# Moving the first tile's pairs three slots later in a two-layer TensorE pipeline

## The reference

```python
h = x @ w_in;   g = h * np.cos(h);        x = g @ w_out            # layer 1
h = np.maximum(x @ w_in2, 0.0);           out = (h * h) @ w_out2   # layer 2
```

## Time and profile before

| | us |
|---|---|
| median of 3 runs | 2253.63 (2253.51 to 2253.69) |
| profiled execution, its own time | 2253.41 |
| its span | 2251.1 |
| TensorE busy | 2239.1 (99%) |
| VectorE busy | 1774.6 (79%) |
| ScalarE busy | 1734.8 (77%) |

### The profile page before, as it was taken

The page is one execution under the profiler, slowest core; times in us unless marked ns, Lnnn a source line. Parts: engine busy times, 40 slices in busy tenths (PEclk is TensorE's granted clock), DMA queues, the critical chain, the costliest instruction groups (busy, mean ns, idle before and its releaser), DMA issues.

```text
span 2251.1 us, 46857 instructions
## 1 busy us (share of the span) xinstructions
PE 2239.1 (99%) x19526; PEld 2213.3 (98%) x19526; DVE 1774.6 (79%) x1813; ACT 1734.8 (77%) x1844; POOL 0.2 (0%) x4
## 2 busy tenths in 40 slices
PE   8999999999999999999999999999999999999999
PEld 7899999999999999999999999999999999999998
DVE  8887788777787777887778877778877788777773
ACT  6677777777877777777778777787777787777876
POOL 0000000000000000000000000000000000000000
PEclk9999999999999999999999999999999999999999
DMA  4000000000000000000000000000000000000000
GB/s 127 27 15 15 9 14 12 10 14 7 14 14 7 14 9 13 14 7 14 14 7 14 14 7 14 7 14 14 7 14 14 7 14 14 7 14 7 7 8 15
DMA packets 13456, 33.26 MB, mean 15 GB/s; under 512 B 1905, under 2 KB 1905, under 8 KB 13169
## 3 DMA queue, kind: packets, MB, share of 16 engines
q1 hardware_dynamic: 13280, 32.81, 4.9%
q10 hardware_dynamic: 144, 0.00, 0.0%
HBM read 20.22 MB, written 12.58 MB: 15 GB/s over the span
## 4 chain that ended last, share of the span: by engine, by line
PE 97%; DVE 2%; ACT 1%; issue 0%; DMA 0%
PE h L346 10%; PE h L350 10%; PE h L348 10%; PE h L352 10%; PE y_A L402 5%; PE y_A L396 5%; PE y_A L400 5%; PE y_A L398 5%; PE y_A L404 5%; PE h L355 5%; PE y_B L400 5%; PE y_B L398 5%; PE y_B L396 5%; PE y_B L404 5%; PE y_B L402 5%; DVE conv L712 0%
## 5 line engine op out<-in xcount | busy, mean ns | idle before, releaser
L698 DVE TENSOR_TENSOR g_lo<-g,g_hi 128x1024 fp32r<-128x1024 f32 x512 | 625.2, 1221 | 272.0 <-ACT g_hi L545 271.1
L545 ACT ACTIVATE g_hi<-g 128x1024 fp32r<-128x1024 f32 x512 | 538.3, 1052 | 44.1 <-DVE g L694 43.4
L537 ACT ACTIVATE w<-w,quarter 128x1024 f32<-128x1024 f32 x256 | 295.5, 1154 | 304.6 <-DVE w L688 304.6
L396 PE MATMUL y_A<-g_hi,dn_lo_A 64*128 64x512 f32 x1024 | 396.9, 388 | 0.1
L402 PE MATMUL y_A<-g_hi,dn_side_A 64*128 64x512 f32 x1024 | 396.3, 387 | 0.0
L398 PE MATMUL y_A<-g_hi,dn_hi_A 64*128 64x512 f32 x1024 | 396.0, 387 | 0.0
L400 PE MATMUL y_A<-g_lo,dn_hi_A 64*128 64x512 f32 x1024 | 395.8, 387 | 0.0
L404 PE MATMUL y_A<-g_lo,dn_side_A 64*128 64x512 f32 x1024 | 395.8, 387 | 0.0
L348 PE MATMUL h<-x_hi_A,up_lo_A 64*128 64x512 f32 x1024 | 394.5, 387 | 0.0
L352 PE MATMUL h<-x_hi_A,up_hi_A 64*128 64x512 f32 x1024 | 394.5, 386 | 0.0
L350 PE MATMUL h<-x_lo_A,up_hi_A 64*128 64x512 f32 x1024 | 394.4, 386 | 0.0
(11 more groups left out here) (122 smaller groups left out, 6180.0 us busy)
## 6 DMA issues: line engine op xcount, KB each, us to landing
xt<-x SPq DMA_DIRECT2D x32, 393.0 KB, 3.1
out<-late SPq DMA_DIRECT2D x32, 256.0 KB, 2.0
out<-late SPq DMA_DIRECT2D x32, 128.0 KB, 2.3
late<-w_out SPq DMA_DIRECT2D x2, 1536.0 KB, 9.5
stage_in_side<-w_in SPq DMA_DIRECT2D x2, 512.0 KB, 4.2
stage_in_side<-w_in SPq DMA_DIRECT2D x4, 256.0 KB, 5.3
w<-w_in SPq DMA_DIRECT2D x1, 768.0 KB, 7.1
stage_in_side<-w_in SPq DMA_DIRECT2D x2, 384.0 KB, 9.1
```

The lines of the kernel that those rows point to most:

```text
L396: mm = pe.matmul(sums[:, 0, :], dn_lo[kind][rows, c, :], hi, start=a, stop=False)
L545: act.activation(g_hi[:, s % RING, :, :], g[:, s % RING, :, :], ACT.Copy).then_inc(hi_made[kind], 1)
L698: dve.tensor_tensor(g_lo[:, r, :, :], g[:, r, :, :], g_hi[:, r, :, :].bitcast(F32), ALU.subtract).then_inc(lo_made[kind], 1)
```

## The change

The first tile's A pairs move from slots 3 to 10 of turn 0 to slots 6 to 13. With the lag of four slots, A6 and A7 of the first tile now go down in slots 0 and 1 of turn 1, in the same slots in which A0' and A1' go up. Turn 1 gets its own table: A0', A1', A2' and then B0', where it was A0', A1', B0', A2'. The read of y_A in turn 1 moves from slot 0 to slot 2 on both ScalarE and VectorE. The taps for the second tile move by two slots, so each stands one A pair earlier; the split of its x is done on ScalarE in slot 13 (that of A7) and on VectorE in slot 15. The low parts of the layer-2 weights get new slots, and those of w_out2 are parted. The fill stays with the down step of A5 and of A6. Down steps of turn 0 all wait for the low part before they begin; A6 and A7, now in turn 1, begin with the high part.

```diff
-FIRST_SLOTS = [("B", 0), ("B", 1), ("B", 2), ("A", 0), ("A", 1), ("A", 2), ("A", 3), ("A", 4),
-               ("A", 5), ("A", 6), ("A", 7), ("B", 3), ("B", 4), ("B", 5), ("B", 6), ("B", 7)]
+FIRST_SLOTS = [("B", 0), ("B", 1), ("B", 2), ("B", 3), ("B", 4), ("B", 5), ("A", 0), ("A", 1),
+               ("A", 2), ("A", 3), ("A", 4), ("A", 5), ("A", 6), ("A", 7), ("B", 6), ("B", 7)]
+SECOND_SLOTS = [("A", 0), ("A", 1), ("A", 2), ("B", 0), ("B", 1), ("B", 2), ("A", 3), ("A", 4),
+                ("A", 5), ("A", 6), ("B", 3), ("A", 7), ("B", 4), ("B", 5), ("B", 6), ("B", 7)]
...
-FIRST_TAP_SLOTS = (4, 5, 6, 7, 8, 9, 10)
+FIRST_TAP_SLOTS = (6, 7, 8, 9, 10, 11, 12)
...
-FIRST_SPLIT_SLOTS, FIRST_LOW_SPLIT_SLOT = (12, 12), 13
+FIRST_SPLIT_SLOTS, FIRST_LOW_SPLIT_SLOT = (13, 13), 15
...
-Y1_SLOT, Y2_SLOT = 0, 3
+Y1_SLOT, SECOND_Y1_SLOT, Y2_SLOT = 0, 2, 3
...
-LATE_AT = {(0, 6): 1, (0, 8): 2, (0, 9): 3, (1, 7): 4}
-LATE_LOW_AT = {(0, 14): 1, (1, 2): 2, (1, 9): 3}
+LATE_AT = {(0, 9): 1, (0, 11): 2, (0, 12): 3, (1, 7): 4}
+
+LATE_LOW_AT = {(0, 15): (1, (0, 1)), (1, 0): (2, (1,)), (1, 3): (2, (0,)), (1, 9): (3, (0, 1))}
...
+        if self.peeled and self.i - back == 1:
+            return SECOND_SLOTS
...
+    def y1_slot(self):
+        return SECOND_Y1_SLOT if self.peeled and self.i == 1 else Y1_SLOT
...
-                return turn.peeled and (turn.i == 1 or turn.i == 0 and p == NP - 1)
+                return turn.peeled and turn.i == 1
...
+                    if turn.peeled and turn.i - back == 0 and made == "A" and runs and q in FILL:
+                        on_zeros(FILL[q])
                     if turn.runs(kind) and runs:
                         up_and_down(turn, s, kind, p, down)
...
-                        if turn.peeled and turn.i == 0 and q in FILL:
-                            on_zeros(FILL[q])
                         down_alone(turn, down)
...
-                    if s == Y1_SLOT and turn.runs("A", 1) and turn.slots() is not LAST_SLOTS:
+                    if s == turn.y1_slot() and turn.runs("A", 1) and turn.slots() is not LAST_SLOTS:
                         read_y1(turn, 1)
...
-                for m, (lo, staged, hi) in enumerate(parts):
-
+                for m in parts_of:
+                    lo, staged, hi = parts[m]
```

More of the change, by code:

```diff
@@ L368, in down_waits @@
                     pe.wait_ge(y2_summed, turn.i - 1)
-                if fine(turn, p):
+                if fine(turn):
                     pe.wait_ge(hi_made[kind], turn.count(kind, p, back))
@@ L372, in down_waits, with fine @@
                     pe.wait_ge(lo_made[kind], turn.count(kind, p, back))
-            def fine(turn, p):
-                return turn.peeled and (turn.i == 1 or turn.i == 0 and p == NP - 1)
+            def fine(turn):
+                return turn.peeled and turn.i == 1
             def down_step(turn, r, kind, p, back, rows, k, first, apart=False):
@@ L388, in down_step @@
                 sums = y["B"] if apart and rows is low and k < 6 else layer_out(turn, kind, back)
-                if fine(turn, p) and k in (2, 7):
+                if fine(turn) and k in (2, 7):
                     pe.wait_ge(lo_made[kind], turn.count(kind, p, back))
@@ L664, in layer1_down_lo, with late_lo_part @@
                                          op1=ALU.subtract).then_inc(late_lo, 1)
-            def late_lo_part(n):
+            def late_lo_part(n, parts_of):
                 if n in (1, 3):
@@ L781, in body @@
                     if turn.peeled and (turn.i, s) in LATE_LOW_AT:
-                        late_lo_part(LATE_LOW_AT[turn.i, s])
+                        late_lo_part(*LATE_LOW_AT[turn.i, s])
             turns(dve, body)
```

## The result

| | before | after |
|---|---|---|
| median | 2253.51 (7 runs, 2252.93 to 2253.70) | 2261.53 (7 runs, 2259.87 to 2262.66) |
| profiled execution, its own time | 2253.41 | 2259.87 |
| its span | 2251.1 | 2258.1 |
| granted clock over the span | 0.999 | 0.997 |

The ratio is 1.0035, with a 95% interval of 1.0024 to 1.0047: the change costs 8.0 us. The forecast was 2259.8 in a range of 2257.0 to 2262.2, slower with a chance of 0.81; the median lies inside the range, 1.7 us above the forecast. Note already here that the profiled execution of the changed kernel is the fastest of its seven; the others took 1.2 to 2.8 us more, where all seven of the kernel before lie within 0.8. The slowest, 2262.66, has a span of 2259.7 like the five at 2261.10 to 2261.74 (2259.3 to 2260.0), so its last 1.1 us lie outside the span.

What follows compares the result with a forecast made beforehand. TensorE, busy 99%, was taken as the bound, with a VectorE-ScalarE ring limiting the stretch before slot 4 of turn 1. Schedule 4.5 + clock 1.7 = 6.2 us on 2253.6 gave 2259.8 us, range 2257.0 to 2262.2.

Steps and rivals of the forecast that it cites:

- Part 1: Taps one A pair earlier: tap 0 ahead of A0's fraction makes everything from there to A6's 0.93 us later.
- Part 2: ScalarE's x split between A7's copy and A6's high part: x1_made at 66.3, a new TensorE wait of 2.3 us.
- Part 3: Slots A0'/A6 and A1'/A7 run from 66.4, done at 75.4; the 18.70 row shows two pairs' matmuls starting together.
- Part 4: Read of y_A behind A1's cosine on ScalarE: B0' waits about 4.3 us for x2_made, slot 4 comes 4.5 us later.
- The sum of the schedule: Start of slot 4 in turn 1 against 82.00, without clock loss: 4.5 us later.
- finish line: Start of slot 4 of turn 1, at 82.00 before; its shift prices the change if no new wait follows.
- Part 5: Granted clock behind the new TensorE waits: 1.7 us lost at the second, 0 at the first (bounds 0 and 1.7).
- Rival C: Both new waits cost the clock: 6.2 + 1.7 us, 2261.5 us; chance 0.18.
- Rival B: No clock lost at either new wait: +4.5 us, 2258.1 us; chance 0.16.
- Rival D: Pairing works, y_A read once A7 is down, B0' input ready: line at 81.2, 2252.8 us; chance 0.11, 0.03 faster.
- milder case: Read of y_A at once at 75.4: x2_made at 78.9, start of slot 4 at 82.4, time 2254.0 us.
- Rival E: VectorE's ring stays behind after slot 4, adding up to 1.5 us: 2261.3 us; chance 0.05.

Runs made afterwards that it cites:

- the read first: Changed kernel with the read and split of y_A one slot earlier (slot 1 of turn 1): 2256.64 us; with zeros in the remaining pauses as well, 2255.29 us.
- the filled kernel: Changed kernel with 16 matmuls on zeros ahead of B0' going up in turn 1 and 16 instead of 8 ahead of A6 going down: 2257.27 us.
- the reordered one: Changed kernel with y_A read in slot 1, x split behind A7's cosine, 14 zeros in first pause, A2' and B0' copies early, larger w2_out part in slot 4: 2254.54 us.
- two reordered kernels: Changed kernel with all causes taken away, 2254.54 us; kernel before with B0' copy ahead of A1' cosine and w_out2 low parts parted, 2253.75 us.

## Why the prediction was right, and where it was off

**Part 1, the shift by a tap.** Foretold 0.93 us for A0 to A6, measured 57.00 against 56.36, which is 0.64. In this execution VectorE took up tap 0 at 20.64, where A0's whole part had begun at 20.92 before; those 0.28 us make up the difference.

**Part 2, the x split.** Foretold: A6's high part 61.5, A7's cosine 62.5, x1_made 66.3, TensorE at 66.4 after a pause of 2.3. Measured: 61.20, 62.17, 66.02, 66.28, 2.46. Right, and 1.0 us of the pause is from the place of the split alone.

**Part 3, the two full slots.** A1' and y_A were foretold for 75.4; the copy that waits for A1' began at 75.26, and the last matmul of y_A had started at 74.78. Two matmuls of different pairs again run side by side out of program order: at 87.92 B1' begins in the upper half, and at 88.33 a step of B0' starts that stands ahead of it in the program. That bears out the row at 18.70, against the rule of strict order in the Trainium skill ("TensorE: Matmul & The Clock Gate", Part 3).

**Part 4, the read of y_A.** Foretold 79.5, 83.0 and 83.1 for the read, x2_made and B0'; measured 79.49, 82.99 and 83.08. The pause was foretold at 4.3 us and measured 4.60, since A2' was up at 78.49 and not 78.8. With the read first B0' goes up at 78.86. (The 84.2 us in that part is when the low part of A0' is made, 84.24 in the trace; slot 4 wants it only when it starts.)

**The sum of the schedule.** Foretold 4.5 us, measured 4.2 with the clock held up. The likely difference is that slot 4's upper half starts ahead of the finish line, while I counted from the half that starts last: with zeros in the second pause the upper half starts 3.8 us later than before (85.77 against 82.00), the lower one 4.7 (86.68), and A3' in slot 6 then goes up 4.2 us later (95.00 against 90.78).

**Part 5, the clock: the term that was mis-sized.** Foretold 1.7 us for the second pause and none for the first. Measured 2.7 for the second, and 1.6 for the first in five of the eleven executions that had only the second filled (in most of the changed kernel's own, by their times). The first size was taken from the row at 31.41, where the clock fell after TensorE had begun again. Behind the second pause it fell at 82.2, ahead of B0', and came back only at 89.0. The length of the rest alone doesn't give the size: behind 2.79 and 2.80 us 1.7 and 2.9 us of work were lost, behind 4.60 and 4.58 us 3.0 and 3.9. It depends on how long before the work the clock falls, and when it comes back, and that differed between executions. A single row therefore gives no price, only one draw. The zero for the first pause was a choice between bounds of 0 and 1.7 us, by the argument that fills run up to it. It was true of the profiled execution; the fills don't protect, as the profiled execution with the read first shows (0.72 over 66 to 72 behind the same fills and the same 2.46 us). The forecast of 2259.8 lies 1.7 us under the median for this reason, and that the profiled execution hit it (2259.87) is luck. Rival C, both pauses charged, gave 2261.5 us, which is where the median lies. Its two clock terms of 1.7 us were 2.7 and 1.6, its schedule of 4.5 was 4.2: the sum is right partly because the two series of runs of the kernel before differ by 0.5 and partly since the errors have opposite signs. "HAM oscillation" in the Trainium skill, the same page, tells of bursts that each start at half clock behind waits of, by its figures, some 3 to 5 us. The second pause (4.60 us) agrees. The first is shorter than those waits, and the runs show that it cost the clock all the same in a part of the executions, as 1.36 us did in one.

**Rival B** (no clock lost) is the filled kernel, 2257.27 against 2258.1; without the zeros it did not occur in any of the seven executions. **Rival D** (the pairing works) is the reordered one: its finish line came at 81.6, foretold 81.2, but the time didn't follow. Its milder case, the read at once at 75.4 and 2254.0 us (0.4 over the kernel before), missed a wait: with the read at 75.26 slot 4 waits for the copy of A2', and the time is 2.1 us over, 1.5 without the surplus of the zeros. The step that failed in it, and in the whole frame for gains, is "nothing on TensorE waits behind 82.00". That is true of the kernel before and says nothing of how near the next wait is; it was within 0.3 us, at the start of turn 2. For a delay the line holds, as the changed kernel shows. For a gain it doesn't. **Rival E** (the ring stays behind after slot 4) did not occur in the changed kernel, which shows no wait there. In the two reordered kernels TensorE does wait for the ring at the start of turn 2, and there the gain is gone.

What stays open: why x1_made of turn 2 comes later in the reordered kernel, which is where its 1.4 us over the kernel before are lost, and what part the small waits near 91 and 118 us have in that; they were seen and not taken away one by one. So it is not shown either whether the pairing as such gains or costs.

## What to carry to other kernels

Moving work of the bottleneck engine beside other work pays only if its inputs come as early; here the paired steps waited for a product of an engine that had to serve a slower chain first. The order on that engine (the read ahead of a cosine, the split behind it) was worth 2.0 and 1.0 us, while no run shows a gain from the pairing. Price a new pause twice, as time and as clock, the clock only where the engine is the bound behind it, and as a range over several executions. Measure it with zeros in it: the filled kernel gives the schedule alone, and its scatter tells whether the clock was in play. A point behind which nothing waits is a sure line for pricing a delay; before a gain is counted on it, look for the next wait that is nearly there.

## What was not expected of the hardware

- A rest of TensorE of 2.46 us left the granted clock at 2.4 GHz in one profiled execution and took it to 1.2 GHz in another (0.72 on average over 66 to 72 us), with the same work around it. The times of a kernel then fall into two heaps 1.6 us apart. A rest of 1.36 us took it down as well in one execution (0.59 over 86 to 90 us).
- Rests of the same length cost different amounts. After 4.60 us the clock was at half for 6.8 us (82.2 to 89.0), 2.96 us of work lost; after 4.58 us in another kernel for some 10.2 us (79.7 to 89.9), 3.9 lost. After 2.79 us it was at 0.57 on average over 4 us, 1.7 lost; after 2.80 us in the changed kernel at half from 31.0 to 37.8, 2.9 lost.
- Those 2.9 us of lost work cost no time, since TensorE waits for other engines in that stretch: 16.58 us from 32.05 to 48.63 with the loss, and 16.58 from 32.17 to 48.75 without.
- With rests filled by zeros, eleven executions of a 2255 us program agree within 0.18 to 0.34 us, so that steps of 1.0 us (0.04%) can be told apart.
